# Two chained MLPs after attention: how 6,016 tokens are cut into pairs of tiles for the second MLP (480 twice against 448 once)

## What is computed

```python
qn = q / (norm(q, axis=1) + 1e-6);  kn = k / (norm(k, axis=1) + 1e-6)
a = softmax(kn.T @ qn / tau)                     # 256 x 256
x = v @ a                                        # 6016 tokens x 256
g = x @ w_gate                                   # d_ff 1536
y = (g * sigmoid(g)) * (x @ w_val) @ w_out       # first MLP
h = y @ w_in2                                    # d_ff 2048
out = (h * clip(h + 3, 0, 6) / 6) @ w_out2       # second MLP
```

## Time and profile before

| | |
|---|---|
| median of 3 runs | 1087.19 us (1087.19 to 1087.28) |
| the profiled execution's own time | 1087.29 us |
| its span, first to last instruction | 1085.5 us |
| PE busy | 1079.9 us, 99% of the span |
| DVE, ACT, POOL busy | 72%, 61%, 30% |
| granted TensorE clock | 1.000, mean over the span |
| start of frame g = 0 (second MLP) | about 591.5 us |

### The profile page before, as it was taken

How to read it: one execution, slowest core, us unless ns; L and a number is a source line. 1 busy time by engine, 2 the same in 40 slices (tenths; PEclk the granted TensorE clock), 3 DMA queues, 4 the chain that set the end, 5 groups by cost and what they waited for, 6 DMA issues and landing times.

```text
span 1085.5 us, 14745 instructions
## 1 busy us (share of the span) xinstructions
PE 1079.9 (99%) x5052; PEld 915.6 (84%) x5052; DVE 781.6 (72%) x1147; ACT 665.7 (61%) x1166; POOL 327.6 (30%) x247
## 2 busy tenths in 40 slices
PE   9999999999999999999999999999999999999998
PEld 7888998888888888888888888998888888888997
DVE  6788779666666766766678777776776776776776
ACT  8731245665665565566577776676676676676654
POOL 7998645200310320223088431220210210210000
PEclk9999999999999999999999999999999999999999
DMA  9711112002102100101122201111111111110111
GB/s 381 249 34 20 40 34 40 1 1 59 20 1 59 21 1 20 40 1 39 59 59 73 78 1 38 22 20 40 18 18 39 20 20 40 20 20 1 21 20 40
DMA packets 111082, 46.83 MB, mean 43 GB/s; under 512 B 91552, under 2 KB 101024, under 8 KB 111008
## 3 DMA queue, kind: packets, MB, share of 16 engines
q1 hardware_dynamic: 110288, 44.58, 15.0%
q10 hardware_dynamic: 720, 1.31, 0.3%
HBM read 33.55 MB, written 12.32 MB: 42 GB/s over the span
## 4 chain that ended last, share of the span: by engine, by line
PE 99%; DMA 0%; DVE 0%; issue 0%
PE psum L1564 47%; PE psum L1586 35%; PE psum L1508 5%; PE psum L1573 4%; PE psum L1518 2%; PE psum L1386 2%; PE psum L1490 2%; PE psum L1418 1%; PE psum L1399 0%; DMA qk_first<-in_k 0%; PE psum L1532 0%; DVE out_sb L445 0%; PE psum L1452 0%; PE psum L1465 0%; PE psum L1474 0%
## 5 line engine op out<-in xcount | busy, mean ns | idle before, releaser
L1586 PE MATMUL psum<-prod,down_w 128*128 128x512 f32 (+1 forms) x1680 | 408.5, 387 | 0.0
L1586 PEld LDWEIGHTS psum<-prod,down_w 128*128 128x128 f32 x1680 | 315.5, 188 | 60.8 <-DVE y_right L1285 0.2
L1564 PE MATMUL psum<-x_even,up_w 128*128 128x512 f32 (+1 forms) x1260 | 302.8, 387 | 0.0
L1564 PEld LDWEIGHTS psum<-x_even,up_w 128*128 128x128 f32 x1260 | 235.5, 188 | 44.4 <-ACT slots L938 0.3
L1564 PE MATMUL psum<-x_odd,up_w 128*128 128x512 f32 x1008 | 245.3, 390 | 0.0
L1564 PEld LDWEIGHTS psum<-x_odd,up_w 128*128 128x128 f32 x1008 | 189.3, 188 | 39.5 <-DVE more_slots L1310 0.4
L1265 DVE TENSOR_TENSOR slots<-psum,slots 128x512 f32<-128x512 f32 (+1 forms) x108 | 74.1, 686 | 123.1 <-ACT slots L946 96.7
L1314 DVE SCALAR_TENSOR_TENSOR prod<-slots,prod 128x512 fp32r<-128x512 f32 (+1 forms) x144 | 100.8, 700 | 32.3 <-ACT prod L989 27.6
L1310 DVE SCALAR_TENSOR_TENSOR slots<-slots 128x512 f32<-128x512 f32 (+1 forms) x120 | 84.1, 701 | 38.0 <-ACT slots L999 38.0
L989 ACT ACTIVATE prod<-slots 128x512 fp32r<-128x512 f32 (+1 forms) x144 | 90.0, 625 | 28.1 <-DVE slots L1310 28.1
L706 POOL TENSOR_TENSOR x_even<-x_even_raw,x_even 128x512 fp32r<-128x512 f32 (+1 forms) x42 | 54.0, 1295 | 159.9 <-ACT x_even L886 159.9
(11 more groups left out here) (149 smaller groups left out, 1308.9 us busy)
## 6 DMA issues: line engine op xcount, KB each, us to landing
out<-out_sb SPq DMA_DIRECT2D x37, 128.0 KB, 2.6
v_in<-in_v SPq DMA_DIRECT2D x36, 128.0 KB, 3.3
qk<-in_q SPq DMA_DIRECT2D x8, 512.0 KB, 9.2
qk<-in_k SPq DMA_DIRECT2D x7, 512.0 KB, 10.6
x_odd_raw<-y_rows SPq DMA_DIRECT2D x12, 256.0 KB, 3.2
y_rows<-act_out SPq DMA_DIRECT2D x10, 256.0 KB, 2.1
y_rows<-y_right SPq DMA_DIRECT2D x10, 256.0 KB, 3.1
down_raw<-in_moe_w_out SPq DMA_DIRECT2D x4, 512.0 KB, 4.0
```

The lines of the kernel that those rows point to most:

```text
L1564: end = mm(bank, w[:, u, k, part, :], XS[pair % 2][:, k, m, 0:pair_width(pair)], start=start and (part, m) == PASSES[0], stop=stop and (pa ...
L1586: end = mm(sums_out(pair_of(f), side, h), w[:, j, part, h * P:(h + 1) * P], buffer_of(f, x)[:, m, :], start=start and (part, m) == PASSES[ ...
```

## The change

The second MLP's pairs 5 and 6 both get 480 tokens a side and hold tokens 0 to 1919 in order; pairs 7 to 10 have 512 a side. Before, pair 6 alone had 448. Four times 480 and eight times 512 are 6,016. A pair's columns are now given by `begin_of`. The pieces of a store are computed from the overlap with the output's tiles: pair 5 has one piece on its left side (tile 0) and three on its right side (tiles 0, 1, 2), pair 6 two on its left (tiles 2, 3) and one on its right (tile 3). The number of stores that `stores_before` expects is summed from the pieces. Both early loads wait for the tiles that were worked alone and for pair 0 of the first MLP.

```diff
-    HALF = (BANK + REST) // 2
+    NARROWER = (3 * BANK + REST) // 4
-    NARROWER, LAST_PAIR = PAIRS + 1, 2 * PAIRS
+    LAST_PAIR = 2 * PAIRS

-    def tile_of(pair, side):
-        if pair < PAIRS:
-            return 2 + 2 * pair + side
-        return 2 + 2 * (pair - PAIRS - (pair > NARROWER)) + side
-
-    def pair_width(pair):
-        return HALF if pair == NARROWER else BANK
+    def pair_width(pair):
+        return NARROWER if PAIRS <= pair < PAIRS + 2 else BANK
+
+    def begin_of(pair, side):
+        if pair < PAIRS:
+            return tokens_at(2 + 2 * pair + side)
+        if pair < PAIRS + 2:
+            return (2 * (pair - PAIRS) + side) * NARROWER
+        return tokens_at(2 * (pair - PAIRS) + side)

         def pieces_of(pair, side):
-            half, full, rest = (n // SQUARE for n in (HALF, BANK, REST))
-            if pair != NARROWER:
-                return ((tile_of(pair, side), 0, 0, full),)
-            return ((0, half, 0, full - half), (1, 0, full - half, rest)) if side else ((0, 0, 0, half),)
+            begin, pieces = begin_of(pair, side), []
+            for n in range(2 + 2 * PAIRS):
+                first = max(begin, tokens_at(n))
+                last = min(begin + pair_width(pair), tokens_at(n) + tokens_of(n))
+                if first < last:
+                    pieces.append((n, (first - tokens_at(n)) // SQUARE, (first - begin) // SQUARE, (last - first) // SQUARE))
+            return pieces

         def stores_before(pair):
-            return 16 * GROUPS * (2 * (pair - PAIRS) + (pair > NARROWER))
+            return 16 * GROUPS * sum(len(pieces_of(p, side)) for p in range(PAIRS, pair) for side in range(2))

             def columns(pair, side):
-                if pair == NARROWER:
-                    return slice(side * HALF, (side + 1) * HALF)
-                at = tokens_at(tile_of(pair, side))
+                at = begin_of(pair, side)
                 return slice(at, at + pair_width(pair))

             def load_y(q):
                 pair = PAIRS + q
                 sp.wait_ge(p3_summed, frames_before(pair - 1))
-                if pair == NARROWER:
+                if pair < PAIRS + 2:
                     sp.wait_ge(y_alone_stored, 64)
+                    sp.wait_ge(y_stored[0], 64)
                 else:
-                    sp.wait_ge(y_stored[q - (pair > NARROWER)], 64)
+                    sp.wait_ge(y_stored[q - 1], 64)
```

More of the change, by code:

```diff
@@ L91, in attention_mlp_mlp_kernel @@
     EPS_NORM, EPS_SUM = 1e-6, 1e-9
-    assert SLOTS < SEGS <= 2 * SLOTS and KC == 2 and 0 < REST < BANK and HALF % SQUARE == 0
+    assert SLOTS < SEGS <= 2 * SLOTS and KC == 2 and 0 < REST < BANK and NARROWER % SQUARE == 0
     assert FIRST + SEGS * SEG == CHUNKS and FRAMES1 % 4 == 0 and FRAMES2 % 4 == 0 and SPLIT.stop == HALVED == SEGS - 2
```

## The result

The median is 1089.66 us (1089.18 to 1090.82, 20 runs) against 1087.53 us for the kernel before in the same runs (1087.19 to 1089.3): ratio 1.0019, 95% interval 1.0013 to 1.0025. The change costs about 2 us. The profiled execution took 1089.18 us with a span of 1087.4, which is 1.9 over that of before. The forecast of 1087.1 was too low, and the median lies beyond the range, which ended at 1089.2.

The account below looks back on a forecast made before the run. The prediction took PE's stream of matmuls, busy 99% of the span, as the bound. Matmuls -0.95 and pair 5's stalls +0.9, all else 0, summed to -0.05 us: 1087.1 us, range 1086.2 to 1089.2.

Parts of the forecast that it names:

- The matmul's price: Pairs 5 and 6: 720 matmuls of 480 columns at 213.3 ns take 153.6 us in place of 154.56, -0.95 us.
- The upper bound: Matmuls of pairs 5 and 6 at 448's overhead, 16.0 ns: 216.0 ns each, 155.5 us for the 720, +0.96 us.
- the prediction's own sign of being wrong: A frame time in pair 6 above 9.74 us, PE idle there, or DVE waiting on a store would refute the prediction.
- 480 streams worse than both neighbours: Rival, every matmul of pairs 5 and 6: from 216.4 ns on, slower; at 226.67 ns the kernel takes 1096.7; chance 0.07.
- The overhead of 448 holds at 480: Rival, matmuls of pairs 5 and 6: 16.0 ns overhead, +0.96 + 0.9, giving 1089.0 us; chance 0.20.
- The straight line: Rival: a 480-column matmul lies between 448 and 512 at 214.67 ns, 0 + 0.9, giving 1088.1 us; chance 0.15.
- Stalls in pair 5: PE's waits for DVE's clip in frames 2, 3 and 4 grow from 0.3 to 1.2 us: +0.9, bounds -0.3 to +1.6.
- Stalls in pair 6: None at 480, since 448 ran the same operations at 9.12 us a frame without waiting; cost 0.
- Queue SP: Stores of pairs 5 and 6 become 28 transfers in place of 20, with nothing due behind them; cost 0.
- The joints: Changes of width at pair 5's start (512 to 480) and pair 7's (480 to 512): two as before, cost 0.
- The sum: Whole kernel: -0.95 + 0.9 = -0.05 us, forecast median 1087.1 us from a median of 1087.19.
- Slower by over 0.2%: Outcome for the whole kernel: a median above 1089.4 us, given a chance of 0.13.

## Why the prediction was wrong

- **The matmul's price was the step that failed.** "With the overhead of 512 (13.3 ns, that of 384 too) a matmul is 213.3 ns" was chosen because three of four widths agree. It measured 216.67. The term was put at -0.95 us and is +1.44, and these 2.4 us are more than the whole miss of the sum. The forecast took 448 for the exception. The stream at 20 widths shows that the four widths in the trace were a thin sample: none of the twelve tried from 508 down to 432 was as low as 13.3, they had 15.0 (500) to 18.7 (456). In that stretch the dear widths are the rule. Why a width has the overhead that it has stays open. The upper bound, 448's 16.0 ns, was also too low by 0.5 us, and the prediction's own sign of being wrong, a frame over 9.74 us in pair 6, came with 9.75; "480 streams worse than both neighbours" had a chance of 0.07, and in kind that is what came, though by 0.7 ns over 448's overhead and not by the 10.7 ns of its upper price.
- **The rivals.** "The overhead of 448 holds at 480", 1089.0 us, came nearest in mechanism and number. Its price row was there, but it got a chance of 0.20 against 0.50. That its number came so near is in part luck: its price was 0.48 us too low and the stalls that it shared with the forecast 0.36 too high. The straight line missed by 1.4 us: 480 isn't on the line between its neighbours. The Trainium skill (TensorE: Matmul & The Clock Gate, section on the back-to-back issue gap) has a fixed part of 2.5 ns beside the columns. The streams here don't agree: over the columns at 2.4 GHz they take 11.7 ns (288 columns) to 18.7 (456) by the width, and 13.3 to 20.0 at 512 columns by the start column.
- **Stalls in pair 5: right in kind and in two of three places, too high in size.** Forecast +0.9 us, measured +0.54. Frame g = 2 had 0.40 for the forecast 0.68, g = 4 0.41 for 0.35, g = 3 none for 0.17, and g = 1, which the forecast left out, 0.06. Part of it is the same error: each matmul came 10.0 ns sooner and not 13.3, so over 48 matmuls 0.48 us and not 0.64; the rest of the 0.28 in g = 2 has no run that explains it. That the stretched clip doesn't get shorter with the width held: 1.32 us against 1.27.
- **Stalls in pair 6: none**, as forecast; every frame there is 9.75.
- **Queue SP: free**, as forecast. The changed kernel issues 16 stores for pair 5 in 26.63 us and the next load a pair later, and no engine waits on a store. The joints cost nothing: right.
- **The sum.** +1.44 + 0.54 = 1.98 against the forecast -0.05; the traces differ by 1.95. The forecast started from a median of 1087.19 in 3 runs, and the 20 runs beside the result have 1087.53, so 0.34 of the 2.56 between 1087.1 and 1089.66 is the start and not the change. "Slower by over 0.2%" had 0.13, from 1089.4 on: the median is above that, but the ratio to the kernel before in the same runs is 1.0019, with an interval on both sides of 1.002. That the change makes the kernel slower is shown, that it does so by over 0.2% is not.

## What to carry to other kernels

Where TensorE is the bound, the price of a matmul against its width is a row to measure before a split is chosen: equal sums of columns were 1.44 us apart here. A narrower stage is only worth its columns while nothing beside it sets the time, so here it belongs behind the stage with the extra casts and not in it. And in this kernel POOL's work had to be placed against DVE's operations with two SBUF operands although POOL itself is 70% idle.

## What the runs showed of the hardware

- The fixed part of a matmul's spacing depends on the width and on the column at which the moving operand starts: 512 columns from 0, 16 and 8 took 226.7, 229.2 and 233.3 ns, 384 took 173.3 from 0 and 176.7 from 8, 448 took 202.7 from 0 and 200.0 from 16, with nothing else running. One PSUM bank in place of eight and one set of weights in place of eight changed neither 448 nor 480; 32 weight columns in place of 128 took 3.2 ns off 480 and 0.4 off 448, and 64 rows in place of 128 added 3.3 to both.
- The same stream took one of two rates in two programs (448: 202.7 or 206.7 ns; 480: 216.7 or 220.0) with its operands at the same addresses, on different chips and behind other stretches, and one program ran at about 1087.5 or 1090.0 us from run to run. What decides it was not found.
- DVE operations with two SBUF operands (480 or 512 columns) that met POOL's instructions took 1.27 to 1.64 us in the places shown, and 0.9 to 1.1 us in some others, instead of 0.65 to 0.69; the clip behind them in the changed kernel, which reads PSUM, kept its 0.64 us beside POOL.
